# Column sums and weight splits of the first step by accumulating transfers, the bias in the second step

## The reference

```python
# x [4, 4096, 192], weight_gen [4, 4096, 8, 7]
w = softmax(weight_gen, axis=-1)              # with 1e-9 added to the sum
x_pad = zero rows (6) ahead of each batch of x
out = einsum('bshk,bskhg->bshg', w, windows of 7 rows of x_pad)   # 8 heads of 24
# then, with x = out as [16384, 192], w_in [192, 2048], w_out [2048, 192], s and b scalars
h = x @ w_in
r = maximum(h, 0)
g = s * (r * r) + b
return g @ w_out
```

## Time and profile before

| | us |
|---|---|
| median of 3 runs | 1158.13 |
| lowest and highest | 1157.95, 1159.02 |
| profiled execution | 1159.53 |
| its span | 1157.6 |
| PE busy | 1143.3 (99%) |
| DVE busy | 901.8 (78%) |
| ACT busy | 770.5 (67%) |
| POOL busy | 119.4 (10%) |

### The profile page before, as it was taken

The page is one execution under the profiler, slowest core; times in us unless marked ns, Lnnn a source line. Parts: engine busy times, 40 slices in busy tenths (PEclk is TensorE's granted clock), DMA queues, the critical chain, the costliest instruction groups (busy, mean ns, idle before and its releaser), DMA issues.

```text
span 1157.6 us, 32334 instructions
## 1 busy us (share of the span) xinstructions
PE 1143.3 (99%) x13348; PEld 1100.3 (95%) x13348; DVE 901.8 (78%) x1164; ACT 770.5 (67%) x843; POOL 119.4 (10%) x74
## 2 busy tenths in 40 slices
PE   7999999999999999999999999999999999999998
PEld 6889999999999999999999999999999999999998
DVE  7888777798777787777887777977778877779744
ACT  4767666666766676666677666767666776666674
POOL 1010111101111101111001111011110011110111
PEclk9999999999999999999999999999999999999999
DMA  7001111011110011110111100111101111101000
GB/s 223 14 28 53 52 52 52 14 38 52 52 52 22 30 52 52 52 52 14 38 52 52 52 30 22 51 52 52 52 14 38 52 52 52 42 21 40 14 15 28
DMA packets 18511, 51.11 MB, mean 44 GB/s; under 512 B 2242, under 2 KB 9793, under 8 KB 18493
## 3 DMA queue, kind: packets, MB, share of 16 engines
q1 hardware_dynamic: 18373, 50.57, 12.6%
q10 hardware_dynamic: 120, 0.28, 0.1%
HBM read 38.25 MB, written 12.58 MB: 44 GB/s over the span
## 4 chain that ended last, share of the span: by engine, by line
PE 96%; DVE 2%; ACT 1%; issue 1%; DMA 0%; SPq 0%; DVEq 0%
PE hp L749 45%; PE op L773 34%; PE op L780 15%; PE hp L680 1%; DVE g_lo L579 0%; DMA x_in<-in_x 0%; ACT r L360 0%; PE op L797 0%; PE hp L686 0%; PE op L696 0%; ACT r L364 0%; DVE g_hi L572 0%; DVE acc L522 0%; DVE wo L542 0%; DVE tap L507 0%
## 5 line engine op out<-in xcount | busy, mean ns | idle before, releaser
L773 PE MATMUL op<-wo,g_hi 64*128 64x384 f32 x4096 | 603.3, 357 | 1.9 <-DVE g_lo L579 0.9
L780 PE MATMUL op<-wo,g_lo 64*128 64x192 f32 x4096 | 560.6, 247 | 0.0
L749 PE MATMUL hp<-xT,w_hi 64*128 64x512 f32 x3072 | 502.4, 390 | 0.5 <-ACT xT L338 0.4
L360 ACT ACTIVATE r<-hp 128x1024 f32<-128x1024 f32 x256 | 257.8, 1019 | 335.3 <-PE hp L749 331.6
L780 PEld LDWEIGHTS op<-wo,g_lo 64*128 64x128 f32 x4096 | 452.0, 188 | 2.1
L773 PEld LDWEIGHTS op<-wo,g_hi 64*128 64x128 f32 x4096 | 445.0, 184 | 5.7 <-DVE wo L542 1.2
L749 PEld LDWEIGHTS hp<-xT,w_hi 64*128 64x128 f32 x3072 | 317.2, 184 | 24.7 <-ACT xT L338 0.6
L579 DVE TENSOR_TENSOR g_lo<-r,g_hi 128x1024 fp32r<-128x1024 f32 x256 | 313.2, 1224 | 31.7 <-ACT g_hi L371 24.8
L749 PE MATMUL hp<-xT,w_lo 64*128 64x512 f32 x1536 | 325.6, 391 | 0.0
L364 ACT ACTIVATE r<-r 128x1024 f32<-128x1024 f32 x256 | 271.0, 1059 | 6.1
L507 DVE TENSOR_TENSOR tap<-x_in,w_soft 128x768 f32<-128x768 f32 x186 | 177.6, 955 | 3.2
(11 more groups left out here) (50 smaller groups left out, 279.8 us busy)
## 6 DMA issues: line engine op xcount, KB each, us to landing
x_in<-in_x SPq DMA_DIRECT2D x30, 960.0 KB, 4.7
out<-out_sb SPq DMA_DIRECT2D x31, 384.0 KB, 2.3
w_in<-in_weight_gen SPq DMA_DIRECT2D x32, 112.0 KB, 2.0
wo_raw<-in_moe_w_out SPq DMA_DIRECT2D x4, 384.0 KB, 5.4
w_raw<-in_moe_w_in SPq DMA_DIRECT2D x4, 256.0 KB, 5.8
x_in<-in_x SPq DMA_DIRECT2D x1, 768.0 KB, 6.7
w_raw<-in_moe_w_in SPq DMA_DIRECT2D x8, 64.0 KB, 5.5
x_in<-in_x SPq DMA_DIRECT2D x1, 384.0 KB, 4.4
```

Of the source, the lines that this page charges most:

```text
L360: nc.scalar.activation(r[:, b, :], hp[:, PAIR * b:PAIR * (b + 1), :], ACT.Relu).then_inc(relu_done, 1)
L749: mm = nc.tensor.matmul(hp[:, j, :], w, xt, start=start, stop=stop)
L773: nc.tensor.matmul(op[:, t, 0:2 * D], g_hi[rows[h], g % 2, j, t * P:(t + 1) * P], wo[rows[h], k, :, :].rearrange("p a d -> p (a d)"), star ...
L780: mm = nc.tensor.matmul(op[:, t, 0:D], g_lo[rows[h], g % 2, j, t * P:(t + 1) * P], wo[rows[h], k, 0, :], start=False, stop=(k == FT - 1 an ...
```

## The change

Everything is in the first step and the beginning of the second. (1) The column sums no longer run on PE. Transfers issued by POOL, four of 384 KB, one for each group of `w_out`, write and then add into `wo_sums`; two more fold its four tiles into one, and 2 matmuls in the transposes of step 0's last second product sum over the partitions. The bias is made in step 1, in banks 2 and 3 of `hp`, and step 1's first product waits for it ahead of its seventh pair. (2) Five of the low parts (`w1` groups 2 and 3, `wo` groups 1 to 3) are no longer a DVE subtraction: ACT writes the negated high part and a transfer issued by POOL adds the weights to it. (3) The first product of the first step begins in another order, and the second half of the transposes goes to `op`, no longer to `hp`. (4) ACT takes over the rounding of one more pair of g, and SP's loads are reordered.

```diff
-            load_wo(2)
+            load_w1(2)
             load_first_x(1)
             load_halo(sp, 1, ((1, 120), (121, 7)))
+            load_wo(2)
+            load_w1(3)
             load_wo(3)
...
-            load_w1(2)
-            load_w1(3)
...
+            def add_w1_to_lo(g):
+                cols = slice(g * GROUP * P, (g + 1) * GROUP * P)
+                half_cols = slice(g * PAIR * P, (g + 1) * PAIR * P)
+                by_parity = moe_w_in[P:D, cols].rearrange("d (m h c) -> d m h c", h=2, c=P)
+                pool.wait_ge(w1_neg_ready, g - 1)
+                pool.dma_start(w1_lo[:, cols], moe_w_in[0:P, cols], accum_op=ALU.add).then_inc(w1_lo_added[g], FETCH)
+                for half in range(2):
+                    pool.dma_start(w2_lo[half * D2:(half + 1) * D2, half_cols].rearrange("d (m c) -> d m c", c=P),
+                                   by_parity[:, :, half, :], accum_op=ALU.add).then_inc(w1_lo_added[g], FETCH)
+
+            def add_wo_to_lo(g):
+                tiles = slice(g * GROUP, (g + 1) * GROUP)
+                pool.wait_ge(wo_neg_ready, g)
+                pool.dma_start(wo[:, tiles, 1, :], w_out_tiles[:, tiles, :], accum_op=ALU.add).then_inc(wo_lo_added[g], FETCH)
+
+            def sum_wo(c):
+                tiles = slice(c * GROUP, (c + 1) * GROUP)
+                if c == 0:
+                    pool.dma_start(wo_sums[:, :, :], w_out_tiles[:, tiles, :]).then_inc(wo_summed, FETCH)
+                    return
+                pool.wait_ge(wo_summed, FETCH * c)
+                pool.dma_start(wo_sums[:, :, :], w_out_tiles[:, tiles, :], accum_op=ALU.add).then_inc(wo_summed, FETCH)
+
+            def fold_sums(c, n):
+                pool.wait_ge(wo_summed, FETCH * c)
+                pool.dma_start(wo_sums[:, 0:n, :], wo_sums[:, n:2 * n, :], accum_op=ALU.add).then_inc(wo_summed, FETCH)
+
+            add_wo_to_lo(1)
             pool.wait_ge(x_halo_loaded[1], 2 * FETCH)
             for q in range(B):
                 zero_batch_start(nc.gpsimd, 1, q).then_inc(pool_zeroed, 1)
                 pool.wait_ge(pool_zeroed, PAIR + q + 1)
+            sum_wo(0)
+            add_w1_to_lo(2)
...
+            fold_sums(NG, 2)
+            fold_sums(NG + 1, 1)
...
-                    if first and q in (3, 5):
+                    if first and q in (1, 3, 5):
                         hi_of_odd_g(q)
                     if first and q == 1:
-                        hi_of_w1(2)
                         hi_of_wo(2)
+                        neg_of_wo(2)
+                    if first and q == 2:
+                        hi_of_w1(3)
+                        neg_of_w1(3)
                     if first and q == 3:
-                        hi_of_w1(3)
                         hi_of_wo(3)
+                        neg_of_wo(3)
...
+            def neg_of_wo(g):
+                tiles = slice(g * GROUP, (g + 1) * GROUP)
+                act.wait_ge(wo_hi_ready, g + 1)
+                nc.scalar.activation(wo[:, tiles, 1, :], wo[:, tiles, 0, :].bitcast(F32), ACT.Copy,
+                                     scale=-1.0).then_inc(wo_neg_ready, 1)
...
             hi_of_wo(1)
+            neg_of_wo(1)
             hi_of_attn_a(0, first=True)
             first_hi_of_attn_b()
             hi_of_w1(1)
+            hi_of_w1(2)
+            neg_of_w1(2)
...
-                taps(1, 1, range(1, 2), FETCH, halo=True)
-                split_g(0, 1, True)
-                bias_of_colsum()
-                lo_of_w1(2)
-                lo_of_wo(1)
-                taps(1, 1, range(2, 5), FETCH, halo=True)
+                split_g(0, 1, True, rounded=True)
+                taps(1, 1, range(1, 5), FETCH, halo=True)
                 split_g(0, 2, True)
                 split_g(0, 3, True, rounded=True)
-                lo_of_w1(3)
-                lo_of_wo(2)
...
+                if second:
+                    bias_of_colsum()
...
-                if second:
-                    lo_of_wo(3)
...
+                    if first and g == 0:
+                        for passes, of_x2 in ((0, 2), False), ((1,), False), ((0, 2), True), ((1,), True):
+                            for j, own, by_x1, by_x2 in banks[:2]:
+                                for n in passes:
+                                    w, xt = by_x2[n] if of_x2 else by_x1[n]
+                                    yield j, w, xt, n == 0 and not of_x2, False
+                        banks = banks[2:]
...
+                    if second and g == 0 and n == 6:
+                        pe.wait_ge(bias_ready, 1)
...
+            def column_sums():
+                for h in range(2):
+                    mm = nc.tensor.matmul(hp[:, 2 + h, PAIR * P:PAIR * P + D], ones[rows[h], :], wo_sums[rows[h], 0, :], start=True, stop=True)
+                mm.then_inc(colsum_ready, 1)
+
...
-                if first or split_now:
-                    pe.wait_ge(wo_lo_ready, g + 1)
+                if first and g == 0:
+                    pe.wait_ge(wo_lo_ready, 1)
+                elif first or split_now:
+                    pe.wait_ge(wo_lo_added[g], FETCH)
...
-                    if first and g == 0 and n == 1:
-                        pe.wait_ge(bias_ready, 1)
...
+                            if first:
+                                pe.wait_ge(wo_summed, FETCH * (NG + 2))
...
-                    if first and g > 0:
-                        pe.wait_ge(w1_lo_ready, g + 1)
-                    first_product(i, g, first)
-                    if first and g == 0:
-                        column_sums(2)
+                    if first and g == 1:
+                        pe.wait_ge(w1_lo_ready, 2)
+                    if first and g > 1:
+                        pe.wait_ge(w1_lo_added[g], 3 * FETCH)
+                    first_product(i, g, first, second)
```

More of the change, by code:

```diff
@@ L93, in mix_and_mlp @@
         first_taps = sb("first_taps", [P, K, STEP, D])
+        wo_sums = sb("wo_sums", [P, GROUP, D])
         scaled_sum = sb("scaled_sum", [P, D])
@@ L130, in mix_and_mlp @@
         wo_lo_ready = sem("wo_lo_ready")
+        wo_summed = sem("wo_summed")
+        w1_neg_ready = sem("w1_neg_ready")
+        wo_neg_ready = sem("wo_neg_ready")
+        w1_lo_added = [sem(f"w1_lo_added{g}") for g in range(NG)]
+        wo_lo_added = [sem(f"wo_lo_added{g}") for g in range(NG)]
         colsum_ready = sem("colsum_ready")
@@ L701, in sum_first_attn @@
                     for h in range(2):
-                        last = nc.tensor.matmul(hp[:, 2 + h, t * D2:(t + 1) * D2], first_taps[rows[h], k, t, D - P:D], ident[rows[h], rows[h]],
+                        last = nc.tensor.matmul(op[:, 2 + h, t * D2:(t + 1) * D2], first_taps[rows[h], k, t, D - P:D], ident[rows[h], rows[h]],
                                                 start=start and t == 0, stop=stop and t == STEP - 1, is_transpose=True)
@@ L708, in _, with first_product @@
                            ((1, True), (3, True), (0, False), (2, False))]
-            def first_product(i, g, first=False):
+            def first_product(i, g, first=False, second=False):
                 def passes_of(h):
-                    w_banks = []
-                    passes = (0, 2, 1) if first and g == 0 else (0, 1, 2)
+                    banks = []
                     for j, own in FIRST_BANKS[h]:
@@ L721, in passes_of @@
                                  (w2_lo[rows[h], f2], xT2[rows[h], 0, :])]
-                        w_banks.append((j, own, by_x1, by_x2))
-                    for j, own, by_x1, by_x2 in w_banks:
-                        some = [by_x1[p] for p in passes] + [by_x2[p] for p in passes if own]
+                        banks.append((j, own, by_x1, by_x2))
+                    if first and g == 0:
[5 more added lines that the diff above has]
+                        banks = banks[2:]
+                    for j, own, by_x1, by_x2 in banks:
+                        some = by_x1 + (by_x2 if own else [])
                         for n, (w, xt) in enumerate(some):
@@ L736, in first_product @@
                         pe.wait_ge(w1_lo_ready, 1)
-                    if first and g == 0 and n == 2:
+                    if first and g == 0 and n == 4:
                         pe.wait_ge(t_lo_ready, 1)
-                    if first and g == 0 and n == 3:
+                    if first and g == 0 and n == 6:
                         pe.wait_ge(t_hi_both_ready, 1)
-                    if first and g == 0 and n == 5:
+                    if first and g == 0 and n == 10:
                         pe.wait_ge(t_lo_both_ready, 1)
+                    if second and g == 0 and n == 6:
+                        pe.wait_ge(bias_ready, 1)
                     if n == 3 and g == 0 and not first:
@@ L749, in first_product @@
                         mm = nc.tensor.matmul(hp[:, j, :], w, xt, start=start, stop=stop)
-                    if n in (5, 11):
+                    if n in ((10, 11) if first and g == 0 else (5, 11)):
                         mm.then_inc(h_bank_left, 1)
```

(9 more changed lines are left out.)

25 lines of the change are left out of this document (16 added, 9 removed).

## The result

The changed kernel takes 1163.68 us (median of 6 runs, 1163.09 to 1165.89) where the kernel before took 1158.22 beside it (6 runs, 1157.95 to 1159.33): ratio 1.0045, 95% interval 1.0035 to 1.0055. It is 5.5 us slower. I had forecast 1153.9, with a range of 1152.0 to 1160.2. The profiled execution took 1165.35 us, its span 1163.3, at a mean granted clock of 0.995. Steps are counted from 0 here, as in the code: the second step, which the prediction calls step 2, is step 1.

What follows compares the result with a forecast made beforehand. PE was taken as the bound, busy 1143.3 of 1157.6 us. Gains of 5.7 us less a 1.5 us wait for POOL's transfers gave 4.2 off 1158.13: 1153.9 us, range 1152.0 to 1160.2.

Steps and rivals of the forecast that it cites:

- Part 1: Step 0's opening: column sums leave PE, first product reordered; group 1 starts at 20.4 instead of 24.15, gain 3.75 us.
- rival C: Step 0's first product: the clock rises only at its end, 2.4 us lost, 1156.3 us; chance 0.07.
- Part 2: Rest of step 0: five splits leave DVE, copies go to ACT; group 3 starts at 39.55, total gain 5.1 us.
- Rival D: Step 0: saved PE time turns into waits for the halo and ACT's copies; gain 1.4 us, 1156.7; chance 0.08.
- Part 3: Step 1's start: bias work hidden, second product waits only 0.2 us; 0.7 us more, total gain 5.7.
- Part 4: POOL's accumulating transfers in step 0: w1 group 3 lands at 41.0, wanted 39.55, so PE waits 1.5 us.
- rival A: POOL's transfer chain in step 0 is longer: wait 5.85 us, 1158.3 us, no change; chance 0.17.
- Rival B: POOL's same transfer chain, slower still: wait 10.5 us with issue 1.5 and landing 6.5, 1162.9 us; chance 0.12.
- the formula: PE's wait ahead of step 0's group 3: 22.7 + 8i + 2L + 2.3 - 39.55, issue i, landing L.

Runs made afterwards that it cites:

- experiment 8: Experiment 7 with w1 group 2's low part back on DVE and its high part on ACT behind the first g: 1155.69 us, 0.9974 of the kernel before.
- experiment 10: Experiment 7 with the kernel before's order of passes in step 0's first product: 1154.83 us, 0.9966 of the kernel before.
- experiment 1: Changed kernel with the column sums' transfers left out, so the bias is zero: 1153.74 us, 0.9954 of the kernel before.
- experiment 5: Changed kernel with SP's 1072 KB of loads for the third step issued only after w1 group 2 landed: 1161.52 us, 1.0020 of the kernel before.
- experiment 7: Changed kernel with the sums behind all low parts on POOL, column sums and bias a step later: 1154.57 us, 0.9963 of the kernel before.
- experiment 6: Changed kernel with 20 and 56 unread matmuls on PE ahead of the waits for w1 groups 2 and 3: 1162.05 us, 1.0024 of the kernel before.
- experiment 12: Experiment 7 run again unchanged: 1154.97 us, 0.9963 of the kernel before.
- experiment 2: Changed kernel with all low parts back on DVE, only the column sums on POOL's transfers: 1160.13 us, 1.0010 of the kernel before.

## Why the prediction was wrong, step by step

**Part 1** was right. First product 14.60 (said 14.9), group 1 at 20.26, released by relu 0 (said 20.4), pairs at 0.23 us. For relu 0 that was in part luck: I had ACT's copies set its time, and in experiment 8, with two of their three pairs gone, it came at the same time, since DVE's part of the softmax was ready no sooner. By their times the clock was up by the transposes of 12.57 (0.46 us for eight, where eight took 0.65 at 10.87), not near 14.4, so rival C did not happen. Too high was only what I gave the new order of the first product by itself: 0.97 us, of which experiment 10 shows 0.3 at most, since relu 0 is late anyway.

**Part 2** was right in size and wrong in one step. The halo landed at 17.4, not 20.7: the accumulation into `wo` group 1 did not hold it up. Then nothing hid that `w1` group 2's transfers must land by 29.7; I had said 29 against 30.75, and they landed at 32.2. The 5.7 us that I gave parts 1 to 3 were 4.9 by the medians with all sums gone (experiment 1), and 5.6 by the two profiled spans (1157.6 and 1152.0). Rival D is answered by that. One small wait was missed: group 2's product waits 0.35 to 0.42 us for a relu where the transfers are in time (experiments 1, 5 and 7).

**Part 3** was right: no engine waits for the bias in step 1, and the second product there starts at 64.73, 4.16 after 60.57, with none of the 0.79 us wait of the earlier trace rows.

**Part 4 failed**, in the landing: "I take 4.0, by the idle rows". It was used for sums 1 and 2, which took 5.3 and 5.4, and by it sum 0 needed no term of its own, while its 10.4 us decided when sum 1 could go. I had `w1` group 3 land at 41.0; it landed at 49.5. The 8.5 us apart are, from the rows of POOL above:
- the halo's memsets ended 3.4 earlier than I said: -3.4;
- from there to sum 1's issue, 11.0 us (19.27 to 30.29) where I had 4.0. I let the four issues decide and took sum 0 as landed by then; it landed at 30.01: +7.0 (with the 6.1 to 7.4 us of other executions it would be +2.7 to +4.0, an estimate);
- sums 1 and 2, 5.6 us each from issue to the next one's issue, not 4.0: +3.2;
- four issues 4.2 us instead of 4.0: +0.2;
- from the last issue's end to the last landing 3.8, not 2.3: +1.5.

The 1.0 us per issue did little harm: the first four took 3.7 us (19.57 to 23.26), the accumulating sums 1.28 to 1.31 each. Of the landing I took a value near the lower end. What spoke for the upper was in my own rows: the `wo` landings of 5.0 to 8.9 were the same bytes into the same kind of tile, and sum 0 had SP's loads beside it. I named the loads under rival A and left them out of the sum. The Trainium skill (DMA: Bandwidth & Descriptors, Anatomy of one DMA) has a fit that gives an estimate of 2.9 us for these bytes. The trace doesn't agree: 3.9 plain on POOL and 5.3 accumulating, issue included (3.2 on SP). Sums 1 to 3 met no rounding on DVE, only additions and subtractions, so they don't test the warning on DVE and POOL's descriptors. The Trainium skill (SBUF — State Buffer, SBUF: two separate sides) says that GpSimd can't write them while DVE is in a two-port operation. The last two issues for `w1` group 2 show something like it: in experiments 6, 7, 10 and 12 they took 2.60 to 2.78 us together where group 3's took 2.32 in 7, and ended 0.1 us behind a rounding on DVE. In the changed kernel they took 2.33, so it cost nothing there.

**Not in the sum at all** is the clock. Behind a wait of 2.59 and one of 6.75 us the next product took 1.6 and 1.5 us more, at the 1.2 GHz level. Experiment 6 shows the cause: with PE at work the same products take 4.13.

The account of the change: at step 1's start the forecast was 50.4 and it was 60.57, 10.2 later. Of these, 8.5 are the later landing of `w1` group 3, 1.5 the clock in the product behind it, and 0.1 or 0.2 small change in the second product. The first wait and its slow product are not in this sum, since PE stood waiting for that landing anyway.

**Rival B** was what happened, in direction: the same chain, slower than before, 1162.9 forecast for it. That its number is near the measured one is in part luck. Its condition (8i + 2L = 22.55) was not met: with i 1.3 and L 5.3 the left side is 21.0, the wait by the formula 6.45 and the time 1158.9, which is rival A's. The first sum, which has no term of its own in the formula, and the clock did the rest.

**Open.** Why sum 0 took 10.4 us in the profiled execution, 3 to 4 more than in others (6.1 to 7.4), isn't settled: the transfers' share is 0.05 from 29 to 30, while it is still pending. The 1.7 us by which that execution is above the median would fit it; no experiment settled it (5 took only the loads away from it, 2 only the transfers for `w1`, and it took 6.5 and 6.1 us; with both beside it, 7.3 to 10.4).

## What to carry to other kernels

A transfer that waits for another one to land holds up every later issue of the same engine: put such a series behind whatever is wanted sooner, and put the use of its result as late as it can go, with a look at what the later use pushes into what (here POOL's additions into a rounding, 1.1 us). Count a series of dependent transfers by its number of landings, each at the figure that the profile shows for as many bytes in the busy stretch, and give the first one its own. Add the clock to each wait of PE of a few microseconds: behind waits of 2.6 to 7 us some 3 us of work ran at 1.2 GHz here, once 5 us. And look for the one landing that decides: a shorter wait ahead of it costs nothing.
